# Top-32 attention, routed experts and a feed-forward layer on one core: the count under the 24th candidate as a sign pass of ScalarE, the ranking one tile further ahead, the attention loop written out

## The reference

```python
scores = scale * np.matmul(q, k.transpose(0, 1, 3, 2))
kth = np.partition(scores, -32, axis=-1)[..., -32:-31]      # 32nd largest of each row
scores = np.where(scores >= kth, scores, -1000000000.0)
attn = softmax(scores); out = np.matmul(attn, v)
```

## Time and profile before

| what | value |
|---|---|
| median of three runs | 1169.23 us (1168.6 to 1170.56) |
| the profiled execution's own time | 1168.81 us |
| its span, first to last instruction | 1166.9 us |
| PE busy | 985.7 us (84%) |
| DVE busy | 794.8 us (68%) |
| ACT busy | 560.7 us (48%) |
| POOL busy | 543.5 us (47%) |
| granted TensorE clock, mean over the span | 0.956 |

### The profile page before, as it was taken

How to read it: one execution, slowest core, us unless ns; L and a number is a source line. 1 busy time by engine, 2 the same in 40 slices (tenths; PEclk the granted TensorE clock), 3 DMA queues, 4 the chain that set the end, 5 groups by cost and what they waited for, 6 DMA issues and landing times. The chain is left out here.

```text
span 1166.9 us, 24330 instructions
## 1 busy us (share of the span) xinstructions
PE 985.7 (84%) x6187; PEld 817.6 (70%) x6187; DVE 794.8 (68%) x3415; ACT 560.7 (48%) x1442; POOL 543.5 (47%) x451
## 2 busy tenths in 40 slices
PE   7888888788877878887593799999999999999995
PEld 4666666666666656665463798888988889888874
DVE  6999989999999999999486333525335253343523
ACT  5877777787777767887241222222122121331211
POOL 4888878787887877888452011111111101441101
PEclk9999989999999989999795799999999999999997
DMA  2101111000111000100352200010000102210000
GB/s 65 32 24 33 33 33 32 11 27 28 32 32 32 17 21 27 32 12 1 118 194 81 99 20 19 20 36 9 27 18 18 36 9 99 65 43 12 20 15 8
DMA packets 38190, 43.48 MB, mean 37 GB/s; under 512 B 24785, under 2 KB 24785, under 8 KB 38098
## 3 DMA queue, kind: packets, MB, share of 16 engines
q1 hardware_dynamic: 34738, 32.06, 8.8%
q0 software_dynamic: 3360, 10.49, 2.7%
HBM read 70.84 MB, written 9.96 MB: 69 GB/s over the span
## 5 line engine op out<-in xcount | busy, mean ns | idle before, releaser
L258 POOL TENSOR_TENSOR rests<-score,work 128x576 f32<-128x576 f32 x144 | 232.5, 1614 | 126.4 <-DVE work L481 126.4
L425 DVE MAX8 cand<-score 128x8 f32<-128x72 f32 x1152 | 215.8, 218 | 9.3 <-ACT score L306 9.3
L536 PE MATMUL bank<-v_sb,prob_t 128*128 128x129 f32 (+1 forms) x1440 | 221.2, 292 | 0.0
L536 PEld LDWEIGHTS bank<-v_sb,prob_t 128*128 128x128 f32 (+1 forms) x1440 | 190.7, 197 | 18.7 <-issue 1.8
L271 POOL TENSOR_TENSOR prob<-prob,rests 128x576 f32<-128x576 f32 x144 | 202.1, 1403 | 0.7 <-DVE rests L485 0.7
L526 PE MATMUL bank<-ident,prob 128*128 128x128 f32 x576 | 98.2, 295 | 108.3 <-POOL prob L271 108.0
L518 PE MATMUL bank<-k_sb,q_sb 64*128 64x288 f32 (+1 forms) x576 | 180.8, 439 | 5.1 <-DMA k_sb<-k_t 4.8
L526 PEld LDWEIGHTS bank<-ident,prob 128*128 128x128 f32 x576 | 63.1, 145 | 172.4 <-POOL prob L271 168.1
L334 ACT ACTIVATE prob_t<-bank 128x512 f32<-128x512 f32 x144 | 86.0, 597 | 102.7 <-PE bank L527 102.3
L518 PEld LDWEIGHTS bank<-k_sb,q_sb 64*128 64x128 f32 (+1 forms) x576 | 102.8, 199 | 27.2 <-issue 6.7
L320 ACT ACTIVATE prob<-score,neg_max 128x576 f32<-128x576 f32 x144 | 110.3, 766 | 0.1
(11 more groups left out here) (177 smaller groups left out, 2139.2 us busy)
## 6 DMA issues: line engine op xcount, KB each, us to landing
raw<-w SPq DMA_DIRECT2D x22, 2048.0 KB
q_sb<-q_t SPq DMA_DIRECT2D x16, 320.0 KB, 3.0
k_sb<-k_t SPq DMA_DIRECT2D x16, 288.0 KB, 3.2
v_sb<-v SPq DMA_DIRECT2D x32, 128.0 KB, 2.3
x_rows<-x_n SPq DMA_DIRECT2D x16, 256.0 KB
win_sb<-w_in SPq DMA_DIRECT2D x1, 2048.0 KB, 8.0
wout_sb<-w_out SPq DMA_DIRECT2D x1, 2048.0 KB, 15.1
v_sb<-v SPq DMA_DIRECT2D x32, 16.0 KB, 2.1
```

The lines of the kernel that those rows point to most:

```text
L258: pool.tensor_tensor(rests[:, s % 2, :], score[:, s % SB, :], work[:, b, :], ALU.mult).then_inc(rested, 1)
L425: ins = dve.max(cand[:, s % 2, 8 * c:8 * c + 8], score[:, s % SB, c * CW:(c + 1) * CW])
L536: last = pe.matmul(out_ps[s % 2], prob_t[0:k, s % 2, c, :], v_sb[par][0:k, c, :], start=(c == 0), stop=(c == KC - 1))
```

## The change

`stage_a` is split. The slow way (`attend_again`) keeps its code and its condition. The fast way becomes `attend_quick`, in which every engine's list is written out for all 144 tiles: there is no loop and no register, and each semaphore is waited on with a constant. In it:

- L481 (`work`, the mask of 576 elements on DVE) and L329 (its sum on ACT) go. DVE writes one element a row, `edge` = 24th candidate times 2^40 (1 - 2^-24). ACT then computes `side` = sign(edge - score times the same constant), -1 from the 24th candidate upwards and +1 below it, with its sum as `balance`.
- POOL's `rest` multiplies scores and `side`. `pick` compares the balance with counts in steps of 2.
- DVE's step t finishes tile t, works the chain of t+2 and takes the chunks of t+3 (before: t+1 and t+2).
- `prob` is 640 wide with zeros from 576 on, so that `turn` makes five pieces of the same size and `save_turned` is one copy of 640 columns.
- The lists of ACT, POOL and PE have a new order.
- `check_quick` reduces 288 columns (thresholds and edges) in place of 16, and looks at the edges' mantissas with five more small DVE instructions.

The diff's core:

```diff
+        # POOL
+            for t in range(2):
+                rest(t, t)
+            for t in range(TILES):
+                mask(t, t % WRAP)
+                if t + 2 < TILES:
+                    rest(t + 2, (t + 2) % WRAP)
...
+        # ACT
+            def take_sides(t, s):
+                act.wait_ge(edge_ready, t + 1)
+                at_least(act, rested, t - 1)
+                at_least(act, picked, t - PB + 1)
+                act.activation(side[:, s % 2, :], score[:, s % SB, :], ACT.Sign, bias=g["edge"][:, t:t + 1],
+                               scale=-EDGE_SCALE, accum_out=balance[:, s % PB:s % PB + 1]).then_inc(sided, 1)
+            def save_turned(t, s):
+                act.wait_ge(turned, t + 1)
+                at_least(act, summed, t - 1)
+                act.activation(prob_t[:, s % 2, :, :].rearrange("p c q -> p (c q)"), turned_ps[:, 0:QW],
+                               ACT.Copy).then_inc(turned_sb, 1)
...
+            for t in range(TILES):
+                if t + 2 < TILES:
+                    take_sides(t + 2, (t + 2) % WRAP)
+                if t + 3 < TILES:
+                    negate_max(t + 3, (t + 3) % WRAP)
+                if t + 2 < TILES:
+                    exp(t + 2, (t + 2) % WRAP)
+                if t >= 2:
+                    save_out(t - 2, (t - 2) % WRAP)
+                if t + 5 < TILES:
+                    save_scores(t + 5, (t + 5) % WRAP)
+                save_turned(t, t % WRAP)
...
+        # DVE, step t (c = t + 2): in place of the mask of 576
+                if chain:
+                    wait_all(dve, (sure_found, c + 1))
+                    dve.tensor_scalar(g["edge"][:, c:c + 1], top[:, jc, SURE - 1:SURE], EDGE, None, ALU.mult).then_inc(edge_ready, 1)
+                if chunks:
+                    candidates(7).then_inc(cand_done, 1)
+                if rest:
+                    wait_all(dve, (picked, t + 1))
+                    dve.tensor_scalar(rests[:, s % 2, :], score[:, s % SB, :], g["thr"][:, t:t + 1], None, ALU.is_ge).then_inc(kept, 1)
...
+        # PE
+            def turn(t, s):
+                pe.wait_ge(masked, t + 1)
+                at_least(pe, turned_sb, t)
+                for c in range(KC):
+                    ins = pe.transpose(turned_ps[:, c * P:(c + 1) * P], prob[:, s % PB, c * P:(c + 1) * P], ident[:, :])
+                ins.then_inc(turned, 1)
+            def values(t, s):
+                pe.wait_ge(turned_sb, t + 1)
+                pe.wait_ge(v_loaded, (t // NT + 1) * 64)
+                at_least(pe, out_saved, t - 1)
...
+            for t in range(6):
+                scores(t, t)
+            for t in range(TILES):
+                if t >= 1:
+                    values(t - 1, (t - 1) % WRAP)
+                if t + 6 < TILES:
+                    scores(t + 6, (t + 6) % WRAP)
+                turn(t, t % WRAP)
+            values(TILES - 1, (TILES - 1) % WRAP)
-            def count(t, s):
-                b = s % PB
-                act.wait_ge(below_ready, t + 1)
-                act.activation(unread[:, :], work[:, b, :], ACT.Copy, accum_out=below[:, b:b + 1]).then_inc(counted, 1)
-                    dve.tensor_scalar(work[:, b_next, :], score[:, j, :], top[:, j, SURE - 1:SURE], None,
-                                      ALU.is_lt).then_inc(below_ready, 1)
```

More of the change, by code:

```diff
@@ L252, in _ @@
         def _(pool):
-            def rest(t, s):
-                b = s % PB
-                pool.wait_ge(below_ready, t + 1)
-                at_least(pool, masked, t - 1)
-                pool.tensor_tensor(rests[:, s % 2, :], score[:, s % SB, :], work[:, b, :], ALU.mult).then_inc(rested, 1)
             def mask(t, s):
                 b = s % PB
[L262 to L268, removed]
+                keeps = score[:, s % SB, :]
+                hold(pool, (ranked, t + 1), (exped, t + 1))
+                pool.tensor_scalar(keeps, score[:, s % SB, :], top[:, s % SB, TOPK - 1:TOPK], None,
+                                   ALU.is_ge).then_inc(kept, 1)
                 pool.wait_ge(kept, t + 1)
@@ L420, in ranked_pair @@
                 dve.sem_clear(rank_step)
[L422 to L457, removed]
-                    left = mark(dve.match_replace(buf, top[:, j, 0:8], buf, NEG))
-                    candidates(2, 3)
-                    hold(dve, (rank_step, left))
-                    best = mark(dve.max(top[:, j, 8:16], buf))
-                    candidates(4, 5)
-                    hold(dve, (rank_step, best))
-                    left = mark(dve.match_replace(buf, top[:, j, 8:16], buf, NEG))
-                if not first:
-                    hold(dve, (rested, t + 1))
-                    next_best = mark(dve.max(top[:, s % SB, SURE:TOPK], rests[:, s % 2, :]))
-                if chain:
-                    hold(dve, (rank_step, left))
-                    sure = mark(dve.max(top[:, j, 16:SURE], buf))
-                candidates(6)
-                if not first:
-                    hold(dve, (rank_step, next_best), (counted, t + 1))
-                    picked = mark(dve.scalar_tensor_tensor(out=pick[:, :], in0=g["counts"][:, :], scalar=below[:, b:b + 1],
-                                                           in1=top[:, s % SB, SURE - 1:TOPK], op0=ALU.is_equal, op1=ALU.mult,
-                                                           accum_out=thr[:, s:s + 1]))
-                if more:
-                    mark(candidates(7))
-                if chain:
-                    hold(dve, (rank_step, sure))
-                    dve.tensor_scalar(work[:, b_next, :], score[:, j, :], top[:, j, SURE - 1:SURE], None,
-                                      ALU.is_lt).then_inc(below_ready, 1)
-                if not first:
-                    hold(dve, (rank_step, picked))
-                    dve.tensor_scalar(rests[:, s % 2, :], score[:, s % SB, :], thr[:, s:s + 1], None, ALU.is_ge).then_inc(kept, 1)
@@ L487, in quick_pair @@
[L487 to L501 removed]
+            def program():
+                all_pairs(dve, ranked_pair)
```

325 lines of the change are left out of this document (242 added, 83 removed).

## The result

The changed kernel takes 1194.54 us (median of 4 runs, 1194.30 to 1195.09) against 1169.08 us before. The ratio is 1.0216, with a 95% interval of 1.0199 to 1.0234: slower, by about 25 us. The forecast was 1187 us with a range of 1163 to 1205.

The account below looks back on a forecast made before the run. PE and ACT in series were to bound the attention at 3.91 us a tile against 3.776: +19.2 us, -1.7 last tiles, -0.3 after the last transpose, +1.4 check, together +18.6 on 1168.81, so 1187 us, range 1163 to 1205.

Parts of the forecast that it names:

- The relay of PE and ACT: Attention, each tile: values wait on ACT's copy of what PE just transposed, in series; 3.06 + 0.70 + 0.15 = 3.91 us.
- The copy: ACT's one copy of 640 columns from PSUM, between transposes and values: forecast 0.70 us a tile.
- The handover from ACT to PE: From the end of ACT's copy to PE's next weight load: forecast 0.15 us a tile.
- PE's own part: From the values' first weight load to the copy's start: 3.34 us with 128-row scores, 3.06 on average.
- The last six periods: Last six tiles, no scores for PE: forecast to fall back to 3.62 us of DVE and POOL, -1.7 us.
- The check: Check after the attention: five more dependent steps of 0.18 us and longer inputs, forecast +1.4 us.
- POOL and DVE in series: Attention: POOL's two products stand between DVE's mask and next pick, excluding DVE; 3.62 us a tile if all else is hidden.
- Rival 1: POOL and DVE bound the attention if PE's gap closes: 3.62 us a tile, some 1148 us, faster; chance 0.09.
- DVE's share: Sign of the forecast: DVE busy only some 85% in the attention, waiting for saved scores or `rests`.
- rival 5: Sign pass fails: table loads in every tile, 1400 us, or attention computed again, more than 540 us on top; chance 0.02.
- rival 4: PE falls to the lower clock level in the attention: +90 us for a fifth of the tiles, 1275 us; chance 0.03.

## Why the prediction was right, and where its terms were off

**The relay of PE and ACT.** This step was right, in place and in kind. Forecast 3.91 us a tile, measured 3.944: four tiles of nine at 3.82, four at 4.03 or 4.04 and the ninth at 4.08. Its parts were less exact than its sum. The copy was put at 0.70 and took 0.703. The handover from ACT to PE was put at 0.15, by a row of the routing, and is 0.05 here (301.14 to 301.19). PE's own part, from the values' first weight load to the start of the copy, was put at 2.92, 3.13 and 3.34 for the three kinds of tile; it is the period less 0.75, so 3.07, 3.28 and 3.33, on average 3.19 in place of 3.06. The 128-row tile, which I had read whole from a stretch without waits, is right to 0.01. The other two I had derived from it by the ends of their score matmuls, and those ends overstate what a short tile saves. From the start of the values to the start of the transposes it is 2.57 us in a 128-row tile and 2.48 (297.16 to 299.64) and 2.27 (301.19 to 303.46) in the two short ones, 0.09 and 0.30 less, where I had 0.21 and 0.42; and the transposes of a short tile take 0.04 us longer to reach the copy. The two errors, +0.13 and -0.10, nearly cancel, and that is luck: the mechanism was read rightly, the closeness of 3.91 to 3.944 was not earned.

**Against the trace, in sum.** From the first copy to the last it is 587.89 - 22.50 = 565.4 us. In the kernel before the same stretch was 560.67 - 21.31 = 539.4, so +26.0, where the sum had +19.2 and -1.7. Three terms of this stretch were off, and they make up 7.9 us. The steady period gives 143 x 0.034 = +4.9. The first two periods were 6.36 and 6.90 us, 5.4 more than the steady ones, in place of 0: PE's work took almost twice as long there, the transposes 1.33 us against 0.77 and nine matmuls of the values 2.60 against 1.46 later.

```profile
21.14 1.33 PE L440 MATMUL bank<-ident,prob 128*128 128x128 f32 x5 [2.17 <-POOL prob L268]
22.50 0.70 ACT L319 ACTIVATE prob_t<-bank 128x640 f32<-128x640 f32 x1 [1.27 <-PE bank L440]
27.50 1.33 PE L440 MATMUL bank<-ident,prob 128*128 128x128 f32 x5
28.86 0.70 ACT L319 ACTIVATE prob_t<-bank 128x640 f32<-128x640 f32 x1 [3.61 <-PE bank L440]
```

Before, slow matmuls at the start lay beside DVE's work (with PE's old order in the changed kernel the first two periods are 3.69 and 4.18 us); in the relay they are on the path. The last six periods, without scores, were 3.07, 3.06, 3.54, 3.61, 3.20 and 3.07 us, 4.1 in all under the steady ones, where I had 1.7 by the 3.62 of POOL and DVE: those two had run ahead and could feed PE for some tiles. Outside this stretch, the first copy starts at 22.50 instead of 21.31, 1.2 us that I had put at 0. From the last copy to the check it is 0.4 us less, where I had 0.3. The check took 1.4 us more, as forecast (2.4 us from its first reduction to its last cast, 1.0 before). The stretch behind it was 2.2 us shorter. Of this, 1.3 us lie between the check's end and DVE's next instruction (5.5 us in place of 6.9); why, stays open. So the sum forecast +18.6 and the span came out at +26.0.

**POOL and DVE in series.** This was right as the second bound: 3.62 forecast, 3.70 measured once PE's order is undone. The term left out is POOL's wait for its own semaphore, 0.14 us; against it, from POOL's end to the next mask it is 0.17 and not 0.10 + 0.14. The reading behind it went further than its rows: they show POOL's product 0.21 us longer (1.61 against 1.40) where the mask overlaps it by 0.35 us, which is not yet a wait for a whole instruction. The runs with picks of 1.10 us and masks of 1.47 us show that. Rival 1 is refuted for the changed kernel and true for the kernel with PE's old order, at 1156 and not 1148 us. The rule of the Trainium skill (SBUF — State Buffer, Who interferes with whom) that a reduction never contends while a two-input instruction and a two-port mode do agrees with the traces: beside POOL's product of 1.41 us the reduction takes 0.14 us, the pick with its two inputs 1.10 (changed kernel) and the mask 1.47 (without the pick). No row shows in which mode the mask runs.

**DVE's share.** I named as a mark of the forecast that DVE would be busy 85% of the attention, and picks of a microsecond as a mark of rival 1. Both were wrong. DVE is busy for 516.83 of 520 us, since a wait for POOL counts as the pick's own time, and DVE's slack in the relay goes into that wait. Only the run without the pick (1193.74 us, no gain) shows that it is slack.

**The rest.** No table was loaded between sign and exponential, and no row of the second attention appears, so rival 5 did not occur; the granted clock in the stretch from 40 to 560 us was 1.00, so rival 4 did not either. The idle time of 2.6 us at the jumps is gone.

## What to carry to other kernels

In an engine's list written by hand, look at what stands between the instruction that produces and the one of the same engine that consumes through another engine: here two moved lines put a copy of 0.70 us and its handovers into the path of every tile, 38 us in all. An engine that is off the path by its busy share (ACT, 47%) can still be on it by its latency; count the loop of waits, not the loads. And when DVE and POOL work on the same tiles, add up the instructions that exclude each other as one resource: shortening one of DVE's others gains nothing while POOL's two products stand in front of the next.

## What the runs showed of the hardware that I had not expected

- An instruction of DVE on nine columns took 0.21 us with POOL idle and 1.10 us with POOL's product running, and the profile counts the wait as busy, not idle.
- A product of POOL that must wait for POOL's previous one starts 0.14 us behind its end; without the wait it starts 0.05 us ahead of the recorded end. That was worth 25.5 us over 144 tiles.
- In the first 30 us the five transposes took 1.33 us in place of 0.77 though the granted clock of the stretches from 10 to 40 us reads 1.00. In the kernel before, the first transposes (1.12 us for four) are as long as those in the stretch from 155 to 160 us, whose granted clock reads 0.50:

```profile
154.93 1.11 PE L526 MATMUL bank<-ident,prob 128*128 128x128 f32 x4 [3.48 <-POOL prob L271]
```

  With the clock at 1.00 the same four take 0.66 us. So by the length of its matmuls PE ran at the pace of the lower level at the start, whatever the clock's row says; that the row is wrong is my reading, no run tests it.
